# Splitting the weights on ScalarE and VectorE, and computing the mish gate of layer two without GpSimd

## The reference, cut to what matters

```
h = x @ w_in1 ; r = max(h, 0) ; g = s * (r*r) + b ; x = g @ w_out1
h = x @ w_in2 ; sp = where(h > 20, h, log1p(exp(min(h, 20)))) ; g = h * tanh(sp) ; out = g @ w_out2
```

## Time and profile before

| | |
|---|---|
| median of 3 runs | 948.8 us (948.29 to 949.64) |
| span of the profiled execution | 947.1 us |
| TensorE busy | 877.8 us (93%) |
| VectorE busy | 662.8 us (70%) |
| ScalarE busy | 370.3 us (39%) |
| GpSimd busy | 235.1 us (25%) |

### The profile page before, as it was taken

How to read it: one execution, slowest core, us unless ns; L and a number is a source line. 1 busy time by engine, 2 the same in 40 slices (tenths; PEclk the granted TensorE clock), 3 DMA queues, 4 the chain that set the end, 5 groups by cost and what they waited for, 6 DMA issues and landing times.

```text
span 947.1 us, 11233 instructions
## 1 busy us (share of the span) xinstructions
PE 877.8 (93%) x4136; PEld 731.1 (77%) x4136; DVE 662.8 (70%) x937; ACT 370.3 (39%) x616; POOL 235.1 (25%) x131
## 2 busy tenths in 40 slices
...
GB/s 215 195 145 43 27 33 38 37 37 37 37 37 37 37 0 1 0 1 1 134 147 75 1 1 1 44 1 1 23 1 1 0 44 0 0 13 32 0 0 44
DMA packets 60639, 36.07 MB, mean 38 GB/s; under 512 B 48320, under 2 KB 50368, under 8 KB 60608
## 3 DMA queue, kind: packets, MB, share of 16 engines
...
## 4 chain that ended last, share of the span: by engine, by line
PE 42%; DVE 20%; issue 19%; ACT 9%; POOL 8%; DMA 1%; SPq 0%; POOLq 0%; ACTq 0%; DVEq 0%
PE Y L792 19%; PE H L778 18%; DVE t L680 6%; POOL g_raw L355 6%; DVE g_raw L688 4%; ACT t L485 3%; DVE g_raw L600 3%; DVE g_raw L691 3%; ACT t L487 3%; DVE g L703 2%; PE H L745 2%; PE Y L806 2%; PE H L766 1%; POOL wout_lo L329 1%; ACT win_hi L390 1%
## 5 line engine op out<-in xcount | busy, mean ns | idle before, releaser
L778 PE MATMUL H<-xs_hi,win_hi 128*128 128x512 f32 (+1 forms) x640 | 241.1, 377 | 9.8 <-POOL win_lo L329 5.4
L778 PE MATMUL H<-xs_lo,win_hi 128*128 128x512 f32 (+1 forms) x640 | 236.7, 370 | 0.0
L778 PE MATMUL H<-xs_hi,win_lo 128*128 128x512 f32 (+1 forms) x640 | 236.6, 370 | 0.0
L806 PE MATMUL Y<-wout_hi,g 128*128 128x512 f32 x576 | 198.9, 406 | 24.3 <-DVE g L703 23.9
L792 PE MATMUL Y<-g,wout_hi 128*128 128x512 f32 (+1 forms) x640 | 188.6, 380 | 14.5 <-DVE g L605 7.3
L355 POOL TENSOR_TENSOR g_raw<-g_raw,t 128x512 f32<-128x512 f32 (+1 forms) x80 | 120.1, 1501 | 297.5 <-DVE g_raw L691 297.5
L600 DVE SCALAR_TENSOR_TENSOR g_raw<-g_raw,s_col 128x512 f32<-128x512 f32 (+1 forms) x80 | 83.5, 1044 | 105.3 <-ACT g_raw L413 105.0
L806 PEld LDWEIGHTS Y<-wout_hi,g 128*128 128x128 f32 x576 | 111.4, 193 | 57.8 <-DVE g L703 34.7
L778 PEld LDWEIGHTS H<-xs_hi,win_hi 128*128 128x128 f32 x640 | 121.6, 190 | 32.5 <-issue 6.2
L792 PEld LDWEIGHTS Y<-g,wout_hi 128*128 128x128 f32 x640 | 119.1, 196 | 34.8 <-DVE g L605 7.8
L778 PEld LDWEIGHTS H<-xs_hi,win_lo 128*128 128x128 f32 x640 | 121.6, 190 | 20.5
...
## 6 DMA issues: line engine op xcount, KB each, us to landing
win_raw<-in_moe_w_in_dram SPq DMA_DIRECT2D x8, 1024.0 KB, 7.5
wout_raw<-in_moe_w_out_dram SPq DMA_DIRECT2D x8, 1024.0 KB, 5.6
...
```

Of the source, the lines that this page charges most:

```text
L778: last = nc.tensor.matmul(Hb[f % banks][:, 0:w], a[:, i, cols], m[:, i, 0:w], start=(i == 0 and n == 0), stop=(i == KC - 1 and n == XPASS ...
L806: last = nc.tensor.matmul(Y[i][:, :], g[:, f % LAG_B, a, rows], m[:, f, :], start=(f == 0 and n == 0), stop=(f == FC - 1 and n == XPASS - 1))
```

## The change

1. **Weight splitting.** GpSimd makes no hi and no lo any more. All hi are made on ScalarE and all lo on VectorE, at fixed steps: in layer one's tile 0 by the tables `FIRST_HI` and `FIRST_LO` (and two lo before that tile), for layer two in tile 4 by `NEXT_HI` and `NEXT_LO`, and the last three in B's first tile as before (`LATE_PARTS`). Tile 0 of A is taken out of its loop on PE, ACT and DVE.
2. **The gate of layer two.** ScalarE takes exp(h) straight from the H bank, one step ahead; VectorE caps it with min(e, e^20) in SBUF, and makes m. With r0 from ScalarE, VectorE computes c = m*r0, a = 2*r0 + c, then (a-2)*c, the refined ratio with its sign turned, and the gate. GpSimd has no part in it. That is seven operations of VectorE in a step where six stood.
3. **Tile ends.** On VectorE the four pieces of the next tile's lo stand between the last operations of the gate (`end_b`), and on ScalarE the next tile's hi stands ahead of the last g hi.

```diff
...
+        SPLIT_ORDER = [(w, layer, i) for layer in range(2) for i in range(NG) for w in ('in', 'out')]
+
+        FIRST_HI = {2: ('out', 1), 4: ('in', 2), 6: ('out', 2), 8: ('in', 3), 10: ('out', 3)}
+        FIRST_LO = {1: ('in', 1), 3: ('out', 1), 5: ('in', 2), 7: ('out', 2), 9: ('in', 3), 11: ('out', 3)}
+        NEXT_HI = {6: ('in', 0), 9: ('out', 0), 10: ('in', 1), 13: ('out', 1), 14: ('in', 2)}
+        NEXT_LO = {7: ('in', 0), 10: ('out', 0), 11: ('in', 1), 14: ('out', 1), 15: ('in', 2)}
         LATE_PARTS = {0: ('out', 2), 3: ('in', 3), 6: ('out', 3)}
...
-            def ratio(T, f, w):
-                pool.wait_ge(r1_done, FC * T + f + 1)
-                t3 = g_raw[:, f % LAG_B, 1, 0:w]
-                nc.gpsimd.tensor_tensor(t3, t3, t1[:, f % 2, 0:w], ALU.mult).then_inc(ratio_done, 1)
...
+                    if isinstance(T, int) and T == 0 and f in FIRST_HI:
+                        kind, i = FIRST_HI[f]
+                        hi_part(kind, 0, i)
+                    if isinstance(T, int) and T == FULL and f in NEXT_HI:
+                        kind, i = NEXT_HI[f]
+                        hi_part(kind, 1, i)
...
             def exp_h(T, f, w):
-                act.wait_ge(min_done, FC * T + f + 1)
-                nc.scalar.activation(t1[:, f % 2, 0:w], t1[:, f % 2, 0:w], ACT.Exp).then_inc(e_done, 1)
+                c = FC * T + f
+                act.wait_ge(h_ready, FC * TILES + c + 1)
+                if f >= 2:
+                    act.wait_ge(ratio_done, c - 1)
+                nc.scalar.activation(t1[:, f % 2, 0:w], Hb[f % HB][:, 0:w], ACT.Exp).then_inc(e_done, 1)
...
+                exp_h(pos, 0, w)
                 for f in range(FC):
-                    exp_h(pos, f, w)
                     rough_inverse(pos, f, w)
+                    if f + 1 < FC:
+                        exp_h(pos, f + 1, w)
                     if f >= 1:
                         g_hi_b(pos, f - 1, w)
...
                 split_hi(TILES + pos + 1, nxt)
+                g_hi_b(pos, FC - 1, width(src))
                 take_rows(pos, src, width(src))
...
+            def lo_part(kind, layer, i):
+                part = slice(i * GF * P, (i + 1) * GF * P) if kind == 'in' else slice(i * GF, (i + 1) * GF)
+                hi, lo, raw = [w[:, :, part] if kind == 'in' else w[:, part, :] for w in (
+                    (win_hi, win_lo, win_raw) if kind == 'in' else (wout_hi, wout_lo, wout_raw))]
+                dve.wait_ge(w_hi, SPLIT_ORDER.index((kind, layer, i)) + 1)
+                nc.vector.tensor_tensor(lo, raw, hi.bitcast(F32),
+                                        ALU.subtract).then_inc(win_ready if kind == 'in' else wout_ready, 1)
...
+                if p == 1:
+                    lo_part('in', 0, 0)
...
+            lo_part('out', 0, 0)
...
-            def min_h(T, f, w):
-                c = FC * T + f
-                dve.wait_ge(h_ready, FC * TILES + c + 1)
-
-                nc.vector.tensor_scalar_min(t1[:, f % 2, 0:w], Hb[f % HB][:, 0:w], 20.0).then_inc(min_done, 1)
-
-            def m_of_e(T, f, w):
+            def min_e(T, f, w):
                 dve.wait_ge(e_done, FC * T + f + 1)
                 t = t1[:, f % 2, 0:w]
+                nc.vector.tensor_scalar_min(t, t, EXP_CAP).then_inc(min_done, 1)
+
+            def m_of_e(T, f, w):
+                dve.wait_ge(min_done, FC * T + f + 1)
+                t = t1[:, f % 2, 0:w]
                 nc.vector.scalar_tensor_tensor(t, t, 2.0, t, ALU.add, ALU.mult).then_inc(m_done, 1)
 
-            def refine(T, f, w):
+            def rough_ratio(T, f, w):
+                dve.wait_ge(r0_done, FC * T + f + 1)
+                t = t1[:, f % 2, 0:w]
+                nc.vector.tensor_tensor(t, t, t2[:, f % 2, 0:w], ALU.mult).then_inc(c_done, 1)
+
+            def unity(T, f, w):
+                dve.wait_ge(c_done, FC * T + f + 1)
+                t = t2[:, f % 2, 0:w]
+                nc.vector.scalar_tensor_tensor(t, t, 2.0, t1[:, f % 2, 0:w], ALU.mult, ALU.add).then_inc(a_done, 1)
+
+            def ratio(T, f, w):
                 c = FC * T + f
-                dve.wait_ge(r0_done, c + 1)
+                dve.wait_ge(a_done, c + 1)
                 if f >= LAG_B:
                     dve.wait_ge(g_used, (FC - 1) * (TILES + T) + f - LAG_B + 1)
+                nc.vector.scalar_tensor_tensor(g_raw[:, f % LAG_B, 1, 0:w], t2[:, f % 2, 0:w], 2.0, t1[:, f % 2, 0:w],
+                                               ALU.subtract, ALU.mult).then_inc(ratio_done, 1)
+
+            def gate(T, f, w):
                 t3 = g_raw[:, f % LAG_B, 1, 0:w]
-                nc.vector.scalar_tensor_tensor(t3, t1[:, f % 2, 0:w], 2.0, t2[:, f % 2, 0:w], ALU.add,
-                                               ALU.mult).then_inc(nr_done, 1)
-                dve.wait_ge(nr_done, c + 1)
-                nc.vector.scalar_tensor_tensor(t3, t3, 2.0, t2[:, f % 2, 0:w], ALU.subtract,
-                                               ALU.mult).then_inc(r1_done, 1)
-
-            def gate(T, f, w):
-                c = FC * T + f
-                t3 = g_raw[:, f % LAG_B, 1, 0:w]
-                dve.wait_ge(ratio_done, c + 1)
+                dve.wait_ge(ratio_done, FC * T + f + 1)
                 nc.vector.scalar_tensor_tensor(t3, t3, -1.0, Hb[f % HB][:, 0:w], ALU.mult, ALU.mult).then_inc(hb_taken, 1)
...
             def tile_b(pos, w):
                 for f in range(FC):
-                    min_h(pos, f, w)
                     if f >= 1:
-                        refine(pos, f - 1, w)
+                        rough_ratio(pos, f - 1, w)
+                    min_e(pos, f, w)
+                    if f >= 1:
+                        unity(pos, f - 1, w)
                     if f >= 2:
                         g_lo_b(pos, f - 2, w)
                     m_of_e(pos, f, w)
                     if f >= 1:
+                        ratio(pos, f - 1, w)
                         gate(pos, f - 1, w)
-                refine(pos, FC - 1, w)
+                    if isinstance(pos, int) and pos == 0 and f in LATE_PARTS:
+                        kind, i = LATE_PARTS[f]
+                        lo_part(kind, 1, i)
+
+            def end_b(pos, w, nxt=None):
+                rough_ratio(pos, FC - 1, w)
+                if nxt is not None:
+                    split_lo(TILES + pos + 1, nxt, [0])
+                unity(pos, FC - 1, w)
                 g_lo_b(pos, FC - 2, w)
+                if nxt is not None:
+                    split_lo(TILES + pos + 1, nxt, [1])
+                ratio(pos, FC - 1, w)
+                if nxt is not None:
+                    split_lo(TILES + pos + 1, nxt, [2])
                 gate(pos, FC - 1, w)
+                if nxt is not None:
+                    split_lo(TILES + pos + 1, nxt, [3])
                 g_lo_b(pos, FC - 1, w)
...
```

More of the change, by code:

```diff
@@ L18 @@
 EPS = 1e-9
+EXP_CAP = math.exp(20.0)
 def linear_attention_moe_kernel(nc, q, k, v, w_in1, w_out1, s, b, w_in2, w_out2, out):
@@ L337, in _ @@
                 q_scale0(Unit(0, p))
-            for i in range(NG):
-                hi_part('in', 0, i)
-                lo_part('in', 0, i)
-                hi_part('out', 0, i)
-                column_max(Unit(1, i))
-                lo_part('out', 0, i)
+            for p in range(NP):
+                column_max(Unit(1, p))
             for batch in range(2, B):
@@ L394, in wout_hi_part, with hi_part @@
                 rows = slice(i * GF, (i + 1) * GF)
-                nc.scalar.activation(wout_hi[:, rows, :], wout_raw[:, rows, :], ACT.Copy).then_inc(w_hi_act, 1)
+                nc.scalar.activation(wout_hi[:, rows, :], wout_raw[:, rows, :], ACT.Copy).then_inc(w_hi, 1)
+            def hi_part(kind, layer, i):
+                (win_hi_part if kind == 'in' else wout_hi_part)(layer, i)
             def split_hi(T, src, x_units=None, parts=range(KC)):
@@ L468, in next_and_take_a @@
                 take_y(KC * T, T, width(T), KC)
-            with act.Fori(0, NEXTRA) as t:
+            tile_a(0, True)
+            next_and_take_a(0, True)
+            with act.Fori(1, NEXTRA) as t:
                 tile_a(t, True)
@@ L531, in k_max @@
                 dve.wait_ge(n.k_in, n.n_in)
-                if not isinstance(n.b, int):
+                if not n.first and not n.fresh:
                     dve.wait_ge(kcol_done, n.u)
```

68 lines of the change are left out of this document (20 added, 48 removed).

## The result

The kernel after takes 901.4 us (median of 4 runs, 899.26 to 903.87) where the kernel before took 948.5 in runs on the same chip: a ratio of 0.950 (95% interval 0.948 to 0.953). The forecast was 895, with a range of 884 to 908. The profiled execution has a span of 901.2, 7.7 more than the 893.5 of the sum; it is one of the longer ones, 903.0 as timed, 1.6 above the median.

The account below looks back on a forecast made before the run. TensorE bounds the kernel but loses 77.0 us to waits and lower clock, mostly from GpSimd's work. With 23.4 left, 53.6 is won: span 947.1 to 893.5, median 1.7 above, so 895; range 884 to 908.

Parts of the forecast that it names:

- the sum: Total over the tile windows: 77.0 us lost before, 23.4 left, 53.6 won, span 947.1 to 893.5.
- lo of `w_in` part 0 ... 0.5: At the start, this lo on VectorE can hold up GpSimd's scaling of q, by 0.5 us.
- A0: Window of layer one's first tile: 18.3 us lost before, 6.7 left after the new weight split.
- the third group of 1.6: In A0, after the waits of up(3) and the kv product, one later group waits 1.6 us.
- A4: Window of layer one's tile 4: 17.0 us lost before, 1.6 left, from held-back pieces of B0's input.
- B0: Window of layer two's first tile: 15.0 us lost before, 5.8 left, mostly up(4) waiting for gate(0).
- 0.3 at the end: Part of B0's remaining loss: 0.3 us at that tile's end.
- B1: Window of layer two's second tile: 10.1 us lost before, 7.0 left, 1 at its start and 6 at its end.
- B2: Window of layer two's third tile: 5.6 us lost before, 0.9 left at the tile's end.
- The boundaries close fully: Rival, chance 0.19: TensorE's slack swallows more of the short waits between tiles; 13 us left, so 885.
- Paid back: Rival, chance 0.17: weight parts queue before gates; at 3.2 to 4.75 a part A0 and B0 lose 12 more, 907.
- Slower: Rival, chance 0.03: layer two's VectorE operations writing the buffer they read are slow; step 7.6 instead of 5.3, 1089 us.

Follow-up runs that it names:

- E8: E1's kernel plus, in each step of layer two, two GpSimd products that nothing reads: 914.7 us.
- E1: The kernel after with one small GpSimd subtraction added as the last instruction of GpSimd's program: 894.3 us.
- E2: The kernel before with one partition_all_reduce added as the last instruction of GpSimd's program: 954.2 us, ratio 1.0071.
- E9: E1's kernel with the three late weight parts at steps 5, 8 and 11 of B0 in place of 0, 3 and 6: 895.5 us.
- E12: The kernel with the edits of E1, E6, E7 and E9, and the three late hi one step ahead of their lo on ScalarE: 880.8 us.
- E6: E1's kernel with the lo of w_out part 0 behind step 0's g lo in A0 instead of ahead of that step: 891.2 us.
- E7: E1's kernel with q's scaling of the first units moved from GpSimd to VectorE: 891.7 us.
- E11: E1's kernel with the min written as a scalar_tensor_tensor of the same buffer twice: 900.5 us.

## Why the prediction was right, and where it missed

**The mechanism was right.** The sum put 54.1 us of gain into waits at named places, less 0.5 for the start; leaving the start out, the profile has 53.3 (947.1 - 901.2 = 45.9, and 7.4 of late start). The agreement is that close because single misses of up to 1.9 cancel. GpSimd's presence was the cause of VectorE's long operations, as the earlier trace rows had it: m falls to 0.684 (forecast 0.69), and E8 brings a good part of the loss back with products that nobody needs. The rival in which writing in place is slow is out: m still writes the buffer that it reads.

**The step that failed** is "lo of `w_in` part 0 ... 0.5", the only cost that the sum gave to the start. I took the rest of it as unchanged because the order of its instructions was. But taking GpSimd out of B changed what its program ends with, and with that what the program finds at its beginning: 7.4 us more (E1, E2), 6.9 more than the sum had, of the 7.7 that are missing. That 0.5 itself came out as 1.6: GpSimd's four scalings take 7.36 from 33.60 on, where four such operations alone take 5.76, because VectorE's lo began at 33.04. In E1, without the late start, less of the lo is left when GpSimd begins, and it is 0.8.

The earlier trace rows held a hint, the 7.37 ascribed to "issue" at 59.09; I read it as GpSimd being late, and didn't ask what the issue was. In A0 of the kernel before GpSimd goes back and forth between weight parts and column maxima, and six such gaps, 40 us in all, stand in its timeline; two of them:

```profile
105.84 0.72 POOL L302 PARTITION_ALL_REDUCE kcol<-kmax  x1 [5.85 <-issue]
...
113.84 4.59 POOL L329 TENSOR_TENSOR wout_lo<-wout_raw,wout_hi 128x2048 fp32r<-128x2048 f32 x1 [7.28 <-issue]
```

The first down's wait of 7.2 us has more of gap ahead of it than of work (7.37, then 4.61). So a part of A0's loss before belongs to these gaps and not to the price of a part on GpSimd, and the new split took both away. No run tells how much each was.

The Trainium skill, "GPSIMD Engine Reference", section "2.1 Instruction dispatch", has a load of about 6 us on the first call of newly loaded code, with no instruction that shows it. The gaps ahead of `partition_all_reduce` (5.6 to 6.4) fit, those ahead of tensor operations (6.6 to 7.8) are longer, and the 9.0 and 10.1 at the start longer still. That a program's end can cause one, that page does not say.

**A0**: forecast 6.7 of loss, measured 4.9. up(3) waited 3.0 (forecast 3.4: it comes 3.2 behind the matmul before it, where 0.2 is usual), the kv product 0.5 (0.9); the third group of 1.6 never came. The half clock that the sum left out behind up(3) did not come here either, but it did in five of the other runs (105.6): that A0 came out below the forecast is in part luck. **A4**: 2.2 for 1.6, 1.2 of it at the place named, the pieces of B0's input, and 0.8 ahead of a down near the end, which was not named.

**B0**: forecast 5.8, measured 7.7. up(4) waited 3.5 (4.1), with 1.7 of half clock (1.4; the granted clock is 0.56 from 502.6 to 506.1). What failed is the "0.3 at the end": downs at the next two late parts waited 0.6 and 1.4, since each of these also makes VectorE stand for its hi (E9, E12). I had counted that wait for the first part alone.

**B1** lost 6.3 (7.0) and left 0.9 of half clock in B2. The same instructions take 50.5 and 87.8 in E1, 49.9 and 87.8 in E6 and E7, so some 2 us of this belong to the one execution that was profiled. **B2** (without the 0.9), **B3** and **B4** are within 0.1. VectorE's step is shorter than forecast, 4.29 for 4.6:

```profile
653.47 0.69 DVE L673 TENSOR_TENSOR t<-t,t 128x512 f32<-128x512 f32 x1
654.08 0.42 DVE L663 TENSOR_SCALAR t<-t 128x512 f32<-128x512 f32 x1
654.41 0.68 DVE L678 SCALAR_TENSOR_TENSOR t<-t,t 128x512 f32<-128x512 f32 x1
...
657.76 0.69 DVE L673 TENSOR_TENSOR t<-t,t 128x512 f32<-128x512 f32 x1
```

Nearly all of that comes from the min, which I priced at 0.61 where its next operation starts 0.33 after it. The price that the forecast had by the Trainium skill, "VectorE: DVE Perf Modes", section "The perf-mode tier table", an estimated 0.42, was right: the trace has 0.423. It was worth more than the 2 us that I gave it: E11 has 6.2, most of it in B0. That it did not show as a gain on the sum is because B0's late parts took it back.

**Rivals.** "The boundaries close fully" is what E12 reaches in B0, but only with another order. "Paid back" came true as to place (A0's and B0's parts in front of gates), at 2.3 a part and not at 3.2 to 4.75. "Slower" set its step of 7.6 against 5.3, but a step can't fall below TensorE's 5.44, so its 147 should have been 138; nothing else hangs on it.
